# The second MLP of a three-stage kernel: block products by Strassen's identity in place of direct ones

## The reference

```
scores = q @ k.T / 8, masked to 0 <= query - key < 64; x = softmax(scores) @ v   # 4 x 8 heads, 576 positions, width 64
x2 = ((x @ w1) * (x @ w2)) @ w3 @ w_out                 # x: 2304 x 512, w1, w2: 512 x 1024, w3: 1024 x 1024, w_out: 1024 x 512
h  = x2 @ w_in;  g = max(0.01 * h, h);  out = g @ w_out2   # w_in: 512 x 2048, w_out2: 2048 x 512
```

## Time and profile before

| | |
|---|---|
| time, median of 3 runs | 843.21 us (843.13 to 843.42) |
| span of the profiled execution | 841.5 us (the profile gives no other time of it) |
| TensorE busy | 829.9 us, 4656 matmuls |
| VectorE, ScalarE busy | 326.9 and 300.3 us |
| GpSimd busy | 38.2 us |
| DMA | 66.19 MB, mean 79 GB/s |

### The profile page before, as it was taken

How to read it: one execution, slowest core, us unless ns; L and a number is a source line. 1 busy time by engine, 2 the same in 40 slices (tenths; PEclk the granted TensorE clock), 3 DMA queues, 4 the chain that set the end, 5 groups by cost and what they waited for, 6 DMA issues and landing times.

```text
span 841.5 us, 12149 instructions
## 1 busy us (share of the span) xinstructions
PE 829.9 (99%) x4656; PEld 781.3 (93%) x4656; DVE 326.9 (39%) x564; ACT 300.3 (36%) x727; POOL 38.2 (5%) x44
## 2 busy tenths in 40 slices
PE   7999999999999999999999999999999999999998
PEld 5789999999999999999999999999999999999997
DVE  5775343443443443443536322322322322322222
ACT  4774433433433433432425222322322322322222
POOL 0110100100100100100000000000000000000000
PEclk9999999999999999999999999999999999999999
DMA  8974232232232232203424002002002002000001
GB/s 282 324 237 151 82 113 88 81 109 89 83 104 89 87 104 90 87 22 130 162 92 158 1 1 76 1 0 76 2 1 75 0 0 75 0 0 31 7 1 38
DMA packets 23067, 66.19 MB, mean 79 GB/s; under 512 B 2560, under 2 KB 5632, under 8 KB 23040
## 3 DMA queue, kind: packets, MB, share of 16 engines
q1 hardware_dynamic: 19584, 61.09, 21.9%
q10 hardware_dynamic: 3456, 4.72, 1.5%
HBM read 56.36 MB, written 9.44 MB: 78 GB/s over the span
## 4 chain that ended last, share of the span: by engine, by line
PE 93%; DMA 2%; DVE 2%; ACT 1%; issue 0%; SPq 0%; ACTq 0%
PE acc L204 20%; PE acc L206 20%; PE acc L205 20%; PE ps_scores L677 4%; PE ps_values L659 3%; PE ps_scores L205 3%; PE ps_turned L206 3%; PE ps_values L205 3%; PE ps_scores L206 3%; PE ps_values L206 3%; PE ps_turned L205 3%; PE ps_scores L204 3%; PE ps_values L204 3%; PE ps_turned L204 3%; PE ps_turned L667 2%; DMA arena<-wprod_tiles 1%
## 5 line engine op out<-in xcount | busy, mean ns | idle before, releaser
L204 PE MATMUL acc<-parts,weights_a 128*128 128x384 f32 x768 | 260.7, 339 | 0.6 <-DVE weights_b L562 0.6
L206 PE MATMUL acc<-parts,weights_a 128*128 128x384 f32 x768 | 258.0, 336 | 0.0
L205 PE MATMUL acc<-parts,weights_a 128*128 128x384 f32 x768 | 257.5, 335 | 0.0
L204 PEld LDWEIGHTS acc<-parts,weights_a 128*128 128x128 f32 x768 | 144.4, 188 | 5.2 <-DVE weights_b L562 1.0
L205 PEld LDWEIGHTS acc<-parts,weights_a 128*128 128x128 f32 x768 | 144.3, 188 | 4.1
L206 PEld LDWEIGHTS acc<-parts,weights_a 128*128 128x128 f32 x768 | 144.1, 188 | 0.0
L625 DVE TENSOR_TENSOR arena<-acc,arena 128x384 f32<-128x384 f32 x96 | 53.5, 557 | 204.1 <-ACT arena L476 204.1
L476 ACT ACTIVATE arena<-acc 128x384 f32<-128x384 f32 x96 | 47.1, 491 | 214.0 <-PE acc L206 214.0
L204 PE MATMUL acc<-weights_b 128*128 128x384 f32 (+1 forms) x256 | 92.9, 363 | 1.7 <-DVE weights_b L502 1.5
L206 PE MATMUL acc<-weights_b 128*128 128x384 f32 (+1 forms) x256 | 89.8, 351 | 0.0
L205 PE MATMUL acc<-weights_b 128*128 128x384 f32 (+1 forms) x256 | 89.7, 351 | 0.0
(11 more groups left out here) (56 smaller groups left out, 976.9 us busy)
## 6 DMA issues: line engine op xcount, KB each, us to landing
arena<-qkm_steps SPq DMA_DIRECT2D x36, 576.0 KB, 3.7
arena<-v_steps SPq DMA_DIRECT2D x36, 256.0 KB, 2.6
arena<-wprod_tiles SPq DMA_DIRECT2D x16, 512.0 KB, 4.1
x_between<-arena ACTq DMA_DIRECT2D x24, 192.0 KB, 1.9
arena<-x_between SPq DMA_DIRECT2D x6, 768.0 KB, 4.3
out<-arena SPq DMA_DIRECT2D x18, 256.0 KB, 2.0
arena<-w SPq DMA_DIRECT2D x8, 512.0 KB, 4.9
arena<-w_in_tiles SPq DMA_DIRECT2D x8, 512.0 KB, 3.5
```

What stands on the lines that cost most here:

```text
L204: eng.matmul(out_ap, w_hi, m_hi, start=start, stop=False)
L205: eng.matmul(out_ap, w_hi, m_lo, start=False, stop=False)
L206: return eng.matmul(out_ap, w_lo, m_hi, start=False, stop=stop)
```

## The change

It replaces both products of the second MLP. Tokens are taken in three chunks of 768 (two of 384, the column halves of the moving factor). Each factor is cut into 2 x 2 blocks, and the product is made with Winograd's form of Strassen's identity: seven block products in place of eight, of sums and differences of blocks.

- Weights come in 16 units: units 0 to 7 hold w_in, 8 to 15 w_out2. A unit is a 128 x 1024 tile of four quarter blocks; GpSimd makes three sums and one more in place (`unit_sums`), so that it holds seven quarters of 256 columns (`UW` = 1792), and ScalarE and VectorE split all seven (`split_unit`). Two staging places are used in turn.
- x2 comes in as four blocks of 768 columns; GpSimd makes four sums (`x2_sums`), ScalarE and VectorE split seven blocks into seven places (`split_x2`).
- The first product is 12 rounds r (3 chunks of 4). A round makes seven products i of two halves s of six matmuls of 384 columns, 84 in all, into six banks: ALPHA for products 0 and 4, BETA for 1, 3 and 6, GAMMA for 2 and 5. ScalarE copies product 0 (`copy_p1`) and c11 (`copy_c11`); VectorE makes u2, u3 and the three other results c22, c12, c21 out of the banks, then the leaky step over three blocks at once (`leaky3`, 1152 columns) and over one (`leaky21`); GpSimd makes the sums of g that the second product needs (`g_sums`, eight of 384 columns a round).
- The seven blocks of g and its sums go from their one staging place (`g_st`) to DRAM (`g_between`), five blocks and then two, for each half (`store_g`).
- The second product takes the seven products of a chunk one after the other, each over eight k-tiles, in 84 block pairs k (three chunks of seven products of four pairs). A pair is loaded from DRAM (`load_t`, 768 columns) and split (`split_t`), up to seven pairs ahead of TensorE; it feeds twelve matmuls of 384 columns, weights stationary. The first four pairs (`TEARLY`) have two places of their own, the others use the space of `g_st`, after everything is stored.
- The output is stored transposed, 512 by 2304, and turned on the host. All rounds are unrolled.

The diff, cut to the order of the work; the sums and the placing of blocks are left out.

```diff
+            def load_unit(n):
+                if n >= 2:
+                    sp.wait_ge(unit_lo, n - 1)
+                src = w_in[n] if n < NPAIR else w_out[n - NPAIR]
+                sp.dma_start(unit_stage(n)[:, 0:4 * QW], src).then_inc(unit_in[n % 2], 16)
+
+            def store_g(r):
+                c, j0 = r // ROUNDS, r % ROUNDS * 2
+                for s in range(2):
+                    sp.wait_ge(gt2_made, 2 * r + s + 1)
+                    sp.dma_start(gt_dram[c, 0:5, :, j0 + s].rearrange("b p t -> p b t"),
+                                 g_st[:, s, 0:5]).then_inc(g_stored[s], 16)
+                for s in range(2):
+                    sp.wait_ge(gt4_made, 2 * r + s + 1)
+                    sp.dma_start(gt_dram[c, 5:7, :, j0 + s].rearrange("b p t -> p b t"),
+                                 g_st[:, s, 5:7]).then_inc(g_stored_late[s], 16)
+
+            def load_t(k):
+                c, i, jp = k // (NPROD * JP), k // JP % NPROD, k % JP
+                if i == 0:
+                    r = c * ROUNDS + jp
+                    for s in range(2):
+                        sp.wait_ge(g_stored[s], 16 * (r + 1))
+                        sp.wait_ge(g_stored_late[s], 16 * (r + 1))
+                if TEARLY <= k < TEARLY + TRAW - SPARE:
+                    for s in range(2):
+                        sp.wait_ge(g_stored[s], 16 * HR)
+                        sp.wait_ge(g_stored_late[s], 16 * HR)
+                if TRAW_BEFORE[k] is not None:
+                    sp.wait_ge(t_lo, TRAW_BEFORE[k] + 1)
+                sp.dma_start(t_raw[traw_slot(k)].rearrange("p (j t) -> p j t", j=2),
+                             gt_dram[c, G_AT[i], :, 2 * jp:2 * jp + 2]).then_inc(t_in[traw_slot(k)], 16)
...
+            for r in range(HR):
+                if r % ROUNDS == ROUNDS - 2 and r // ROUNDS + 1 < NC2:
+                    sp.wait_ge(unit_lo, NPAIR)
+                    sp.wait_ge(xs_lo, NPROD * (r // ROUNDS + 1))
+                    load_x2(r // ROUNDS + 1)
+                if r == HR - ROUNDS:
+                    sp.wait_ge(xs_lo, NPROD * NC2)
+                    for n in range(2):
+                        load_unit(NPAIR + n)
+                if r == HR - 1:
+                    for k in range(SPARE):
+                        load_t(k)
+                if r > HR - ROUNDS:
+                    for n in range(2):
+                        load_unit(NPAIR + 2 * (r - HR + ROUNDS) + n)
+                if r == HR - 1:
+                    for k in range(SPARE, TEARLY):
+                        load_t(k)
+                store_g(r)
+            for k in range(TEARLY, TB):
+                load_t(k)
...
+            def x2_sums(c):
+                pool.wait_ge(x2_in, 32 * c + 32)
+                pool.tensor_tensor(extra, y12, y11, ALU.subtract).then_inc(t1_made, 1)
+                pool.wait_ge(t1_made, c + 1)
+                pool.tensor_tensor(y12, y22, y12, ALU.subtract).then_inc(t3_made, 1)
+                pool.wait_ge(xs_lo, NPROD * c + 1)
+                pool.tensor_tensor(y11, y22, extra, ALU.subtract).then_inc(t2_made, 1)
+                pool.wait_ge(xs_lo, NPROD * c + 3)
+                pool.wait_ge(t2_made, c + 1)
+                pool.tensor_tensor(extra, y21, y11, ALU.subtract).then_inc(t4_made, 1)
+
...
+            for r in range(HR):
+                if r == 0:
+                    unit_sums(HALF_UNITS)
+                    unit_sums(HALF_UNITS + 1)
+                if r == 1:
+                    unit_sums(HALF_UNITS + 2)
+                    unit_sums(HALF_UNITS + 3)
+                if r % ROUNDS == ROUNDS - 1 and r // ROUNDS + 1 < NC2:
+                    x2_sums(r // ROUNDS + 1)
+                if r >= HR - ROUNDS:
+                    for n in range(2):
+                        unit_sums(NPAIR + 2 * (r - HR + ROUNDS) + n)
+                g_sums(r)
+
...
+            for r in range(HR):
+                copy_p1(r)
+                more = r % ROUNDS == ROUNDS - 1 and r // ROUNDS + 1 < NC2
+                if r > HR - ROUNDS:
+                    for n in range(2):
+                        split_unit(NPAIR + 2 * (r - 1 - HR + ROUNDS) + n)
+                if r < 2:
+                    split_unit(HALF_UNITS + 2 * r)
+                if more:
+                    for i in range(4):
+                        split_x2(r // ROUNDS + 1, i)
+                if r == HR - 1:
+                    for k in range(SPARE):
+                        split_t(k)
+                copy_c11(r)
+                if r < 2:
+                    split_unit(HALF_UNITS + 2 * r + 1)
+                if more:
+                    for i in range(4, NPROD):
+                        split_x2(r // ROUNDS + 1, i)
+                if r == HR - 1:
+                    for k in range(SPARE, TEARLY):
+                        split_t(k)
+            for n in range(2):
+                split_unit(2 * NPAIR - 2 + n)
+
...
+            def make_c22(r):
+                for s in range(2):
...
+                    dve.wait_ge(u2_done, 2 * r + s + 1)
+                    dve.tensor_tensor(u3_sb[:, s], banks[BETA + s][:, 0:CT], u2_sb[:, s], ALU.add).then_inc(u3_done, 1)
+                    dve.wait_ge(u3_done, 2 * r + s + 1)
+                    if 0 < r < HR:
+                        dve.wait_ge(g_stored[s], 16 * r)
+                    elif r > HR:
+                        dve.wait_ge(out_stored[3], 16 * (r - HR))
+                    dve.tensor_tensor(place_c(r, s, 1, 1), banks[GAMMA + s][:, 0:CT], u3_sb[:, s],
+                                      ALU.add).then_inc(c22_done, 1)
...
+            for r in range(HR):
+                make_u2(r)
+                more = r % ROUNDS == ROUNDS - 1 and r // ROUNDS + 1 < NC2
+                late = r > HR - ROUNDS
+                if late:
+                    split_unit(NPAIR + 2 * (r - 1 - HR + ROUNDS))
+                if more:
+                    split_x2(r // ROUNDS + 1, 0)
+                make_c22(r)
+                if late:
+                    split_unit(NPAIR + 2 * (r - 1 - HR + ROUNDS) + 1)
+                if more:
+                    for i in range(1, 3):
+                        split_x2(r // ROUNDS + 1, i)
+                if r == HR - 1:
+                    for k in range(SPARE):
+                        split_t(k)
+                for s in range(2):
+                    make_c12(r, s)
+                    leaky3(r, s)
+                if more:
+                    split_x2(r // ROUNDS + 1, 3)
+                if r == HR - 1:
+                    split_t(SPARE)
+                for s in range(2):
+                    make_c21(r, s)
+                    leaky21(r, s)
+                if more:
+                    for i in range(4, NPROD):
+                        split_x2(r // ROUNDS + 1, i)
+                if r < 2:
+                    for n in range(2):
+                        split_unit(HALF_UNITS + 2 * r + n)
+            for k in range(SPARE + 1, TEARLY):
+                split_t(k)
...
+            def bank_waits(r, i, s):
+                n = 2 * (r - 1) + s + 1
+                if i == 0:
+                    if r == 0:
+                        pe.wait_ge(masked, NSTEP)
+                        pe.wait_ge(pt_done, NSTEP)
+                    else:
+                        pe.wait_ge(c11_done, n)
+                if i == 1:
+                    if r > 0:
+                        pe.wait_ge(c21_done, n)
+                    elif s == 0:
+                        pe.wait_ge(xa_done, NSTEP)
+                        pe.wait_ge(xb_done, NSTEP)
+                    else:
+                        pe.wait_ge(acc_free, 4 * HALVES + KM * (NCH - 1) + 1)
+                if i == 2:
+                    if r == 0:
+                        pe.wait_ge(acc_free, 4 * HALVES + KM * (NCH - 1) + 2 + s)
+                    else:
+                        pe.wait_ge(c12_done, n)
+                if i == 3:
+                    pe.wait_ge(u2_done, n + 2)
+                if i == 4:
+                    pe.wait_ge(p1_copied, n + 2)
+                if i == 5:
+                    pe.wait_ge(c22_done, n + 2)
+
```

More of the change, by code:

```diff
@@ new lines, in _ @@
+            x2_sums(0)
+            for n in range(HALF_UNITS):
+                unit_sums(n)
+            for r in range(HR):
[11 more added lines that the diff above has]
+                g_sums(r)
@@ L784 @@
+            for r in range(HR):
+                first_product(r)
+            for c in range(NC2):
+                second_product(c)
 def kernel(q, k, v, moe_w1, moe_w2, moe_w3, moe_w_out, moe2_w_in, moe2_w_out):
```

558 lines of the change are left out of this document (345 added, 213 removed).

## The result

The changed kernel takes 889.34 us (median; 888.33 to 889.83) against 843.17 for the kernel before on the same chip, a ratio of 1.0554 with the interval 1.0539 to 1.0569. It is 46 us slower; 835 was forecast, with a range to 855. The profiled run took 888.33 us, 1.8 above its span of 886.5; before, the difference was 1.7.

What follows compares the result with a forecast made beforehand. TensorE's matmul stream was taken as the bound, moved only by columns or holes. Terms -50.0 + 1 + 6.5 + 11 + 7.5 + 11.5 + 4 + 0.4 = -8.1 gave a span of 833.4, forecast 835 us, range 813 to 855.

Steps and rivals of the forecast that it cites:

- tail: End of the second MLP: two sums and a larger store in place of a copy and store, 0.4 us more.
- (b) to (e): Stalls taken in rounds 0 and 1 (6.5 us), 3 and 7 (11), 9 and 10 (7.5), and at the hand-over (11.5).
- free order: Each stall worked out with neither GpSimd nor VectorE held by the other; taken values lie between this and strict.
- slow pace: TensorE's matmuls run at half pace after long holes: 4 us taken, between 2 and 8.
- rival B: GpSimd and VectorE don't hold each other, free values everywhere: 24.6 us of stalls against 52.4 of gain, 815 us; chance 22%.
- entry, rounds 0 and 1: Unit splits ahead of u2 and stores queued behind a unit load: free 4.5 us, strict 8.0, taken 6.5.
- token exchange: Rounds 3 and 7, where the next 768 tokens come in: free 2 us each, strict 9 each, taken 5.5 each.
- late rounds: Rounds 9 and 10, two output weight units each, GpSimd's unit sums ahead: free 5.0 us, strict 9.5, taken 7.5.
- hand-over: Start of the second product, only four block pairs ready before the last store: free 8.7 us, strict 16, taken 11.5.
- strict: Each stall worked out with each operation of GpSimd or VectorE waiting out one of the other.
- Its sign for them: VectorE's leaky step well over 1.36 us, or GpSimd's sums over 0.78, would show the turns.
- Rival C: GpSimd and VectorE take strict turns, mainly in rounds 3 and 7 and the hand-over: 58.9 us of stalls, 852; chance 28%.
- Rival D: Stores of five blocks land more than 3 us later than forecast, all 11 round changes stall: 846 us; chance 8%.

Runs made afterwards that it cites:

- g6: Changed kernel with every two-input SBUF instruction of VectorE in the second MLP reading its second input from an unused PSUM bank, values wrong; 849.85 us.
- g1: Changed kernel with every GpSimd sum of the second MLP cut to 32 columns, all waits kept; 821.93 us.
- g4: Changed kernel with 274 extra TensorE matmuls into a bank nobody reads, ahead of the long waits; 888.68 us.
- i1: Changed kernel with all 172 GpSimd sums of the second MLP moved to VectorE at full size; 874.67 us.

## Why the prediction was wrong

The gain in matmuls, 50.0, measured 52.4. Plain rounds, the second product and the tail cost what was said, stores and VectorE's lengths too. The kinds of stall were named; their sizes were wrong.

**The failed step** is the pricing of the stalls, (b) to (e), and it failed in two places, first of all in the free order. With nobody held they were to cost 24.6 us, slow pace and tail included (rival B); in g6, where nobody is held, they cost 59.8 (us over pure):

| stall | forecast, free | g6 | g1 |
|---|---|---|---|
| entry, rounds 0 and 1 (measured to 2) | 4.5 | 11.7 | 9.9 |
| token exchange | 4 | 10.9 | 2.6 |
| late rounds | 5.0 | 19.4 | 4.4 |
| hand-over | 8.7 | 17.8 | 14.5 |

g1's 31 us are near the forecast in sum, though entry and hand-over were too low even so: the free order fits GpSimd sums that cost nearly nothing. What it left out is how GpSimd's sums delay loads and stores in rounds with other work, above all the ring of load, unit sums, g sums, store and c22. It was seen only as "GpSimd's sums for it go in front".

The second place is the choice of "a value between" free and strict turns. They are strict in both directions. Its sign for them came, too: the leaky step's mean is 1.64 us and the g sums' 1.13 to 1.56. Their price was forecast well, 34 us between B and C against 39 measured; by the prediction's own sums the choice cost 17 us. Rival C was the case in kind, and at 852 still 37 short, because it stood on the same free order. (C's sum also takes 1 for the entry where its strict value was 3.)

**GpSimd's length** was scaled from one row, the 1.04 of a sum of 512 columns with a broadcast second input, to 0.78 for 384. It is 1.01: 2.16 ns a column and about 0.2. The alternative in the text, 0.91, would have been nearer. The 28 us between g6 and g1 are the price of the whole length; what the missing 0.23 us a sum cost by themselves no run shows.

**The stalls by term**, each against what was taken. Entry with rounds 0 to 2: 18.5 against 7.5. Token exchange: 24.7 against 11, of which the holes proper are 19.0 (C has 18); the 21 us of shared work that it names are 23 by its own lengths. Late rounds: 29.2 against 7.5 for two of the three, and 9.5 in strict order, the term most wrong. Hand-over: 25.4 against 11.5. The last store lands 26.5 us after round 11's last matmul (682.3 to 708.8), where strict order had 19.6: the unit's load stands behind stores and pair loads on SyncE's queue, the eight unit sums begin only at 682.5, and the g sums at 693.1. Loads were taken too short as well, a weight unit's at 3.8 for 5.1, x2's at 4.3 for 6.8. The slow pace, 4 in the sum, is contained in these numbers (22 us); g4 shows for 8 of them that they cost nothing of their own. So -52.4 - 1.5 + 18.5 + 24.7 + 29.2 + 25.4 + 0.7 + 0.3 gives +45 us of span.

Rival B fell: 815 against 849.9 in g6. Rival D fell as well: 4.1 us for the stores, and no stall in plain rounds.

## What to carry to other kernels

When a change removes matmul columns by adding elementwise sums, add up the new work per round on each helper engine with lengths measured at that very width, and where GpSimd and VectorE both read two SBUF inputs, add the two together; if a round with extra duties exceeds its matmul time, at least the excess comes out (here GpSimd's 14.0 and VectorE's 7.8 us are 21.8 in turns against 14.6; the late rounds took 22.8 to 26.0). That each engine's work fits is not enough: with no turns GpSimd's 14.0 fit under 14.6, and the late rounds still took 18.5 to 23.2 us (g6). Look for rings, too: a buffer's store, behind sums, behind a load, behind that same store; add up the times around the ring and compare them with the round. In these runs, moving work earlier or reordering it paid only where the place that it went to had slack.

## What the runs showed of the hardware

A GpSimd sum of 32 columns takes 0.25 us, of 256 0.74, 384 1.01, 768 1.85; VectorE needs 0.55 for 384 and 0.42 for 256. These are lengths with nobody beside (g6, g1, i1). A 32-column sum behind a split took 1.97 us, until the whole split was over (g1): it was not slowed, it waited its turn. With one input of VectorE's instruction from PSUM both sides are free at unchanged length (VectorE 1354 and 2012 ns, GpSimd 1014; g6). In the changed kernel matmuls of 384 columns stand 0.1733 us apart at a granted clock of 1.00 (750 to 850 us) and 0.32 at 0.50 (446 to 449 us, behind a hole of 3.7).
